# Turned weights in three banks instead of two, and the output products in one piece

## The reference, cut to what matters

```
scores = q @ k.T / 8, causal, softmax -> a          # per head, 576 x 576
local  = a @ v
mem    = (phi(q) @ M_prev) / (phi(q) @ z_prev)
x      = g * mem + (1 - g) * local                   # 2304 tokens x 512
h      = x @ w_in;  u = h * softmax(h)               # 2304 x 1024
y      = layer_norm(u) * g_ln @ w_out                # 2304 x 512
out    = (sigmoid(y @ w_gate) * (y @ w_val)) @ w_out2
```

## Time and profile before

| what | value |
|---|---|
| median of three runs | 867.9 us (866.55, 867.9, 868.19) |
| the profiled execution's own time | 869.41 us |
| its span, first to last instruction | 867.4 us |
| PE busy | 835.6 us, 96% |
| DVE busy | 604.6 us, 70% |
| ACT busy | 463.8 us, 53% |
| mean granted clock of PE | 0.994 |

### The profile page before, as it was taken

How to read it: one execution, slowest core, us unless ns; L and a number is a source line. 1 busy time by engine, 2 the same in 40 slices (tenths; PEclk the granted TensorE clock), 3 DMA queues, 4 the chain that set the end, 5 groups by cost and what they waited for, 6 DMA issues and landing times.

```text
span 867.4 us, 14377 instructions
## 1 busy us (share of the span) xinstructions
PE 835.6 (96%) x5224; PEld 699.9 (81%) x5224; DVE 604.6 (70%) x1464; ACT 463.8 (53%) x958; POOL 38.5 (4%) x47
## 2 busy tenths in 40 slices
PE   5888899999999999998999999999999999999998
PEld 3565677777777777876888999999999999999997
DVE  7887886667777766387674677688666668766653
ACT  6766665666555654355254444465444456444443
POOL 1000000010000000021000000000000000000000
PEclk9999999999999999999999999999999999999999
DMA  6241111111011100100122311113011112211102
GB/s 196 71 155 45 43 43 41 31 43 43 17 43 44 43 16 15 49 2 0 41 58 73 122 49 50 48 50 121 28 48 50 50 50 85 86 49 39 34 1 74
DMA packets 62166, 46.56 MB, mean 54 GB/s; under 512 B 6544, under 2 KB 52624, under 8 KB 62096
## 3 DMA queue, kind: packets, MB, share of 16 engines
q1 hardware_dynamic: 62096, 45.64, 17.1%
HBM read 40.91 MB, written 4.72 MB: 53 GB/s over the span
## 4 chain that ended last, share of the span: by engine, by line
PE 90%; DVE 5%; issue 2%; ACT 2%; DMA 0%; POOL 0%; SPq 0%; DVEq 0%; ACTq 0%
PE tt_bk L1485 10%; PE tt_bk L1483 10%; PE tt_bk L1484 10%; PE m_bk L1364 9%; PE s_bk L1388 7%; PE tt_bk L1298 5%; PE s_bk L1245 4%; PE o_bk L1306 4%; PE s_bk L1535 3%; PE s_bk L1536 3%; PE s_bk L1534 3%; PE o_bk L1388 3%; PE m_bk L1535 2%; PE s_bk L1364 2%; PE m_bk L1536 2%
## 5 line engine op out<-in xcount | busy, mean ns | idle before, releaser
L1485 PE MATMUL tt_bk<-xc_hi,wc_lo 128*128 128x384 f32 x476 | 160.0, 336 | 0.0
L1483 PE MATMUL tt_bk<-xc_hi,wc_hi 128*128 128x384 f32 x476 | 159.9, 336 | 0.0
L1484 PE MATMUL tt_bk<-xc_lo,wc_hi 128*128 128x384 f32 x476 | 159.8, 336 | 0.0
L564 ACT ACTIVATE p_nat<-p_nat,negmax 128x512 f32<-128x512 f32 (+2 forms) x144 | 82.9, 577 | 72.3 <-DVE negmax L872 72.3
L1089 DVE TENSOR_TENSOR wc_lo<-wc_raw,wc_hi 128x768 fp32r<-128x768 f32 x72 | 78.3, 1088 | 31.8 <-ACT wc_hi L629 31.8
L1483 PEld LDWEIGHTS tt_bk<-xc_hi,wc_hi 128*128 128x128 f32 x476 | 89.4, 188 | 6.1
L1484 PEld LDWEIGHTS tt_bk<-xc_lo,wc_hi 128*128 128x128 f32 x476 | 89.4, 188 | 6.1
L1485 PEld LDWEIGHTS tt_bk<-xc_hi,wc_lo 128*128 128x128 f32 x476 | 89.4, 188 | 0.0
L872 DVE CUSTOM_DVE_ANT_0 p_nat<-s_bk,mask 128x384 f32<-128x384 f32 (+2 forms) x124 | 54.9, 489 | 28.3 <-PE s_bk L1245 27.9
L629 ACT CAST wc_hi<-wc_raw 128x768 fp32r<-128x768 f32 x72 | 64.4, 944 | 0.1
L1298 PE MATMUL tt_bk<-ident,p_nat 128*128 128x128 f32 x400 | 56.8, 280 | 7.9 <-ACT pT L571 7.6
(11 more groups left out here) (211 smaller groups left out, 1807.8 us busy)
## 6 DMA issues: line engine op xcount, KB each, us to landing
wc_raw<-in_moe_w_val SPq DMA_DIRECT2D x36, 256.0 KB, 3.0
wc_raw<-in_moe_w_gate SPq DMA_DIRECT2D x36, 256.0 KB, 3.4
qkT<-in_q SPq DMA_DIRECT2D x16, 288.0 KB, 2.9
qkT<-in_k SPq DMA_DIRECT2D x16, 288.0 KB, 3.2
v_raw<-in_v SPq DMA_DIRECT2D x16, 256.0 KB, 2.8
out<-o_sb SPq DMA_DIRECT2D x15, 256.0 KB, 2.2
w_raw<-in_moe_w_out SPq DMA_DIRECT2D x12, 256.0 KB, 4.6
xT<-in_moe_w_in SPq DMA_DIRECT2D x1, 2048.0 KB, 9.6
```

What stands on the lines that cost most here:

```text
L564: nc.scalar.activation(p_tile(g, tile), p_tile(g, tile), ACT.Exp, bias=negmax[:, n:n + 1], scale=-1.0, accum_out=den[:, n:n + 1]).then_inc ...
L1483: mm(o, hi[:, k, c, :], xc_hi[:, j, c, :], start=start and c == 0, stop=False, skip_group_check=True)
L1484: mm(o, hi[:, k, c, :], xc_lo[:, j, c, :], start=False, stop=False, skip_group_check=True)
L1485: last = mm(o, lo[:, k, c, :], xc_hi[:, j, c, :], start=False, stop=c == 1, skip_group_check=True)
```

## The change

In steps with tiles (pairs g-1 = 4 and later) fills rotate through three banks, `t_bk[1]`, `t_bk[0]` and `o_bk`. A fill n of 3 or more waits for the copy of fill n-3; fill 2 waits for `x_ok`. The order on PE changes: fills 0 to 2 stand between the second and the third piece of hidden products, fills 3 to 5 behind the third, then twelve output products in one piece, then fill 6. The order on ACT, DVE, POOL and SP is the same; the copies read the bank that `turn_bank` names. The early steps use the two banks as before, with the same waits.

```
--- before.py
+++ after.py
@@ -207,6 +207,13 @@
         def p_tile(g, tile):
             return p_nat[g % 2][:, p_at[tile]:p_at[tile] + keys(tile)]
 
+        def turn_bank(g, n):
+
+
+            if g < M0 - 1:
+                return t_bk[1 - n % 2]
+            return (t_bk[1], t_bk[0], o_bk)[n % 3]
+
         def tail_bank():
             return m_bk[:, 0, 0:P]
 
@@ -568,7 +575,7 @@
                 act.wait_ge(pt_filled, NF * g + n + 1)
                 wait(act, o_ready, 2 * g)
                 c = P * len(FILLS[n])
-                nc.scalar.copy(pT[:, 512 * n:512 * n + c], t_bk[1 - n % 2][:, 0:c]).then_inc(pt_act_ok, 1)
+                nc.scalar.copy(pT[:, 512 * n:512 * n + c], turn_bank(g, n)[:, 0:c]).then_inc(pt_act_ok, 1)
 
             def keep_x(h, n):
                 act.wait_ge(o_ready, 2 * h + n + 1)
@@ -915,7 +922,7 @@
                 dve.wait_ge(pt_filled, NF * g + n + 1)
                 wait(dve, o_ready, 2 * g)
                 c = P * len(FILLS[n])
-                nc.vector.tensor_copy(pT[:, 512 * n:512 * n + c], t_bk[1 - n % 2][:, 0:c]).then_inc(pt_dve_ok, 1)
+                nc.vector.tensor_copy(pT[:, 512 * n:512 * n + c], turn_bank(g, n)[:, 0:c]).then_inc(pt_dve_ok, 1)
 
             def split_w1(c):
                 dve.wait_ge(w1_hi_ok, c + 1)
@@ -1286,14 +1293,18 @@
 
             def turn_p(g, n):
                 pe.wait_ge(p_ok, NB * g + max(order.index(tile) for tile, _ in FILLS[n]) + 1)
-                if n < 2:
-                    if g >= M0 - 1:
+                if g >= M0 - 1:
+                    if n < 2:
                         pe.wait_ge(memo_ok, 2 * g + 2 - n)
-                    elif g:
-                        copied(g - 1, NF - 1 - n)
-                else:
+                    elif n == 2:
+                        pe.wait_ge(x_ok, 2 * g)
+                    else:
+                        copied(g, n - 3)
+                elif n > 1:
                     copied(g, n - 2)
-                bank = t_bk[1 - n % 2]
+                elif g:
+                    copied(g - 1, NF - 1 - n)
+                bank = turn_bank(g, n)
                 for c, (tile, j) in enumerate(FILLS[n]):
                     last = nc.tensor.transpose(bank[:, c * P:(c + 1) * P],
                                                p_nat[g % 2][:, p_at[tile] + j * P:p_at[tile] + (j + 1) * P], ident[:, :])
@@ -1434,19 +1445,15 @@
                 if g < PAIRS:
                     scores(g, 2)
                 moe_hidden(t, 12, 18)
-                turn_p(g - 1, 0)
-                turn_p(g - 1, 1)
+                for n in range(3):
+                    turn_p(g - 1, n)
                 moe_hidden(t, 18, 24)
-                turn_p(g - 1, 2)
-                turn_p(g - 1, 3)
+                for n in range(3, 6):
+                    turn_p(g - 1, n)
                 if t:
                     if g < PAIRS:
                         pe.wait_ge(max_ok, NU * g + NU - 1)
-                    moe_out(t - 1, 0, 6)
-                turn_p(g - 1, 4)
-                turn_p(g - 1, 5)
-                if t:
-                    moe_out(t - 1, 6, 12)
+                    moe_out(t - 1, 0, 12)
                 turn_p(g - 1, 6)
                 if g < PAIRS:
                     scores(g, 3)
```

## The result

The changed kernel took 870.35 us (median of 20 executions), the kernel before 867.82 us (20 executions beside it). Ratio 1.0033, 95% interval 1.0024 to 1.0042: some 2.9 us slower. The forecast was 868.2 us, the range ended at 870.0 us.

What follows compares the result with a forecast made beforehand. PE was taken to bound the kernel, busy 835.6 of 867.4 us. Terms: 0 (pieces) + 0 (waits) + 0.3 us (t = 0) = +0.3 us, so 868.2 us on the median's scale; range 866.2 to 870.0 us.

Steps and rivals of the forecast that it cites:

- Pieces, 0 us: PE, t = 1 to 11: one change from blocks to products fewer per step gains 0; at most 1.0 us.
- New waits in t = 1 to 11, 0 us: PE's fills 2, 3, 5 and 6 in ordinary steps: waits for x_ok or copies never show, 0 us.
- Hidden row 0.44 us later, absorbed in t = 1 to 11: Four blocks of fill 2 delay the hidden row's maximum 0.44 us per step; 1.59 us of cover makes it free.
- Step t = 0, +0.44 us on the dependency: Last hidden product, hence norm and turned rows, 0.44 us later; the freed 1.06 us of waits become idle time later.
- the 2.4 us piece: End of t = 0: PE idles 2.4 us in one piece before the next scores, where it was 1.07 us.
- The clock gives back 0.13 us: Behind t = 0: 1.2 GHz stretch at 95.1 to 98.5 us stays, PE works 0.26 us less in it, -0.13 us.
- Rival C: End of t = 0: longer idle piece brings a second or prolonged 1.2 GHz stretch, +2.0 us, 869.9 us; chance 9%.
- A: Changes between blocks and products cost 0.09 us each, part of t = 0's waits gained: -1.0 to -2.0 us; chance 9%.
- B: The slow clock stretch at 95.1 us behind t = 0 vanishes: -1.3 us, 866.6 us; chance 5%.
- D: Every step: the later hidden row reaches PE, 12 x 0.44 = +5.3 us, 873.2 us; chance 2%.

Runs made afterwards that it cites:

- with the clock held: Added blocks keep PE busy in all long idle places: kernel before 864.86 us, change in t = 1 to 11 only 865.15 us, whole change 865.71 us.
- Experiment 4: Changed kernel, but fill 2 behind the last six hidden products (7, 15, 3 blocks): 870.06 us, ratio 1.0033 against the kernel before.
- Experiment 6: Kernel before, with 8 and 7 added blocks keeping PE busy in two idle places at the end of t = 0: 867.39 us, ratio 0.9997.
- experiment 2: Kernel before, with new order and third bank in step t = 0 only: 870.2 us, ratio 1.0035 against the kernel before.
- experiment 3: Changed kernel with three banks but the old order of pieces (7, 7, 8, 3 blocks): 867.98 us, ratio 1.0011 against the kernel before.

## Why the prediction was wrong

- *Pieces, 0 us*: right in kind. A seam less gains nothing, and the steps even got 0.02 to 0.03 us longer each, 0.29 us in all with the clock held, beyond the bound of 0.1 us that I had set. Why they did is open.
- *New waits in t = 1 to 11, 0 us*: right; copies and third bank were in time. Experiment 4 shows how near the edge is: with fill 2 behind the hidden products, in one piece with fills 3 to 5, fill 5 waits.
- *Hidden row 0.44 us later, absorbed in t = 1 to 11*: right, cover 1.60 us.
- *Step t = 0, +0.44 us on the dependency*: right, 0.45 us in the trace and 0.56 us with the clock held. That the freed waits turn into idle time later was right too, down to the 2.4 us piece (2.25).
- *The clock gives back 0.13 us*: this step failed, and it carries nearly all of the miss. It has the wrong sign and size: about 2.0 us lost (2.9 less 0.85). I took the stretch at 95 us in the one profiled execution for a fixture of the kernel, to be moved a little. Experiment 6 and the table of clocks show that it is a matter of chance, absent in part of the executions of the kernel before. After the change low clock came more often: 2 of 28 executions at 0.996 or higher, where it had been 60 of 96.
- *Rival C*, priced at +2.0 us and 869.9 us, was nearest. Right in it was that the idle time in one piece brings more stretches onto work; but it asked for a second stretch beside a sure first one, and that is seen in experiment 2 only, while both profiles of the changed kernel have one there, as before. I gave it 9% because "most of the earlier stretch would hold little work". The stretches in the profiles lie behind the idle piece, where the work is. Its price lay inside the range; it was too low, since the clock cost 2.0 us instead of 1.7 and the path 0.85 us instead of 0.3. That the result missed the range by only 0.35 us says nothing for the forecast.
- *Rivals A, B and D*: no gain at the seams, no vanished stretch, no delay by the norm in the ordinary steps.

Open: how often each single stretch comes. One execution of each kernel (two of the changed one) has its clock over time; of the others only the mean is known. The mean is a coarse measure: on one chip, at 0.996 the changed kernel takes 868.5 us (2 executions) and the kernel before 867.3 (12), at 0.992 they take 871.2 (5) and 869.0 (3), more apart than the 0.85 us of the path. That a stretch falls on work in one case and not in the other would explain it, but was not tested. Experiment 2 and the changed kernel lose more clock (0.9925, 0.9928) than experiment 3 (0.9936); they have the third wait, 0.67 us, in addition, but that this is the reason was not tested. How much of the clock loss lies in a second stretch in a row, as in the profile of experiment 2, is open too, and so is how much in the tail: the stretch near 397 us is in the profiles of the changed kernel (twice) and of experiment 4, and in none of the other six with that idle time.

## What to carry to other kernels

Where PE stands idle, ask not only whether a wait is on the path but how the idle time is distributed after the edit: here 3.04 us in four pieces became 3.90 us in three, the path grew by 0.45 us and the time by 2.9. The clock in one profile is a sample; compare the mean granted clock over all executions before it goes into a sum, and get the price of a stretch from distances on PE or from a kernel with its idle places filled. Where an idle piece of 2 us can't be removed, filling it with work that nobody needs can pay, and it also makes small differences between kernels measurable.

## What the runs showed of the hardware

- Stretches of about 3.4 us at 1.2 GHz follow idle pieces of PE of 2.0 to 2.3 us in part of the executions, here near 23, 66, 94 and 397 us (in two profiles behind two pieces of 1.07 and 0.91 us); one more of them in an execution is 0.002 of mean clock. On work it costs 1.6 us, read in two places; the one near 15 us, with all places filled, cost nothing that could be measured.
- With turned blocks of the identity in the idle places of t = 0, PE stays at 2.4 GHz there, and the mean clock is 0.9963 instead of 0.9928.
- A wait of 0.17 us can leave no idle row on PE, because a block is shown 0.27 us long and so reaches over it. Only the distances between starts show it.
